# Routing each token tile inside the delta rule, and the experts as a pipeline over tiles

## The chip, the cores and the metric

The kernel runs on one core of a Trainium2 chip. The metric is the device time of one execution in microseconds; the median of three runs is compared. The core has five engines that each take their instructions in order: TensorE (PE; its weight loads are shown as PEld), VectorE (DVE), ScalarE (ACT), GpSimd (POOL) and SyncE (SP, which here only issues DMAs). They meet through semaphores. 16 DMA engines move the data.

## The reference, cut to what matters

Three layers follow each other: a delta-rule attention over 32 heads (4 batches of 8) with 768 time steps, a mixture of eight experts in which every token goes to one, and a dense layer with three input matrices.

```
for t in range(S):                                   # delta rule, S = 768, D = 48
    y[:, :, t] = einsum('bhd,bhde->bhe', q[:, :, t], state)
    v_old = einsum('bhde,bhd->bhe', state, kt)
    state = state + bt * einsum('bhd,bhe->bhde', kt, vt - v_old)
...
e_idx = argmax(x @ w_gate)                           # x: 3072 tokens x 384
for e in range(8):
    mask = e_idx == e
    out[mask] = gate_w * eom * (relu(x[mask] @ w1[e]) @ w2[e])      # 384 -> 1024 -> 384
...
h = maximum(maximum(x @ w1, x @ w2), x @ w3)         # 384 -> 768
out = h @ w_out
```

## The kernel before

The program is a row of blocks, each with one instruction stream per engine.

**Delta rule** (`attention_and_router`). The tokens are 24 tiles of 128 rows: 12 steps k, each with two streams st = 0 and 1 that are worked on side by side. A step is cut into 16 slots, and `walk` writes out by hand, for every engine, what it does in each slot: `CHAIN` is the recurrent part of a step (ks, z, up for each half, then yt and lg: turn the tile round and make its router logits), `INV` is the preparation of a later step (turn the keys, gram, an inversion in levels), `PRE` and `NORM` the normalisation of keys. Stream 1 runs 9 slots behind stream 0. `run` walks w from -1 to 13: in it, a is the step under preparation (k = w), c the step in the chain that began an iteration before, b the one before that, n the next one whose keys are normalised. So four steps are in flight. A bank of PSUM per stream (`chain`) holds all of CHAIN's results; two others and a third (`bank`) those of INV.

The names that matter below: POOL makes `ksq` (NORM part 0), `kn` and `beta_mask` (PRE), `n_lo` ("low") and `n_kb_a` ("kb", which reads the keys in `k_own`); in slot yt it copied the finished tile into `x_all`. SP runs `load_k(k + 1)` and then `load_qv(k)` for each k:

```
for k in range(2, STEPS):
    if k + 1 < STEPS:
        load_k(k + 1, (k + 1) % 2)      # k_raw x2, then k_own x2; k_own of stream st waits for kb_ready[st] >= k
    load_qv(k, k % 2)                   # kq_t and v_in of stream 0, then of stream 1; wait for state_out
```

TensorE's gram of step k and stream 0 (slot 1 of iteration w = k) waits for `qv_in`, that is for kq_t and v_in of this step.

**Routing** (`route_and_sort`). After the last tile, VectorE picks each token's expert from the logits of all 24 tiles at once, TensorE counts (rank of a token among those of its expert), VectorE makes slots and the table of expert ranges, and POOL scatters the 24 tiles with an indirect DMA each into `x_sorted`. The weights of expert 0 are split there in a high and a low part (float32r).

**Experts** (`experts`). 28 tiles of sorted tokens; for each, TensorE does the first layer ("hidden", 18 matmuls of 512 columns into `h_bank`), turns the next tile's x (`transpose_x`, L838), turns h (L859), and does the second layer (24 matmuls of 384 columns into `y_acc`), each engine in a loop from the expert's first tile to its last. VectorE makes the next expert's high parts at an expert's start (`before`), POOL the low parts.

**Last layer** (`last_layer`). Six blocks of 512 tokens; rows are gathered from `y_sorted` with an indirect DMA.

Of the kernel before, what the change touches and what calls it, by code (L numbers as in the profile page):

```python
# [10 lines left out]
I32 = mybir.dt.int32  # L11
# [28 lines left out]
CF_TRI = CF_BASE + C  # L40
CF_ONE = CF_TRI + P
CF_IOTA = CF_ONE + P
CF_STEP = CF_IOTA + E
CF_SUM = CF_STEP + TILES
CF_END = CF_SUM + E * E

# [3 lines left out]
CH_END = CH_REP + U * C  # L50


def constants():
# [11 lines left out]
    cf[:, CF_TRI:CF_TRI + P] = np.arange(P)[:, None] < np.arange(P)[None]  # L65
    cf[:, CF_ONE:CF_ONE + P] = 1.0
    cf[:, CF_IOTA:CF_IOTA + E] = np.arange(E)
    cf[:, CF_STEP:CF_STEP + TILES] = P * np.arange(TILES)
    cf[:, CF_SUM:CF_SUM + E * E] = np.tri(E).reshape(-1)
    ch[:, CH_ID:CH_ID + P] = np.eye(P)  # L70
    ch[:, CH_NEG:CH_NEG + P] = -np.eye(P)
    ch[:, CH_REP:CH_REP + U * C] = np.tile(row == col, (1, U))
    return cf, ch
# [22 lines left out]
def attention_and_router(nc, ctx, sems, kt_in, kh, qh, vh, bh, cf_in, ch_in, wr_in, cf, ch, wr, x_all, logits, xs, ys, xs_zeroed, weights, w1, w2):  # L96
# [36 lines left out]
    y_tile = single("y_tile", [P, X], F32)  # L133
    y_t = single("y_t", [P, KX, P], F32)
    zeros = sb("zeros", [P, X], F32)

# [41 lines left out]
    x_out = pair_of("x_out")  # L178
# [11 lines left out]
    ident_rep = ch[:, CH_REP:CH_REP + U * C]  # L190
    LV0, LVS = 2, LEVELS - 2
# [44 lines left out]
    def _(sp):  # L236
# [24 lines left out]

        sp.wait_ge(zeros_ready, 1)
        with sp.Fori(0, MAXB + 1) as g:
            sp.dma_start(xs[bass.ds(P * g, P), :], zeros[:]).then_inc(xs_zeroed, 16)

        with sp.Fori(TILES, MAXB + 1) as g:
            sp.dma_start(ys[bass.ds(P * g, P), :], zeros[:]).then_inc(xs_zeroed, 16)

# [3 lines left out]
        for k in range(2, STEPS):  # L272
            if k + 1 < STEPS:
                load_k(k + 1, (k + 1) % 2)
            load_qv(k, k % 2)

    @block.tensor
    def _(pe):
# [83 lines left out]
        def chain(k, par, st, what, e):  # L362
            out = yb[st]
            W = 2 * D
            if what == "ks":
# [4 lines left out]
                elif k >= 1:  # L370
                    pe.wait_ge(logit_out[st], k)
# [24 lines left out]
            elif what == "yt":  # L396
# [3 lines left out]
                for c in range(KX):  # L400
                    ins = pe.transpose(out[:, P * c:P * c + P], y_tile[st][:, P * c:P * c + P], ident)
# [863 lines left out]
```

## Time and profile before

| | us |
|---|---|
| median of 3 runs | 1198.79 (1197.86 to 1202.87) |
| profiled execution, its own time | 1203.62 |
| span of the profiled execution | 1201.9 |
| PE busy | 1030.9 (86% of the span) |
| DVE, ACT, POOL busy | 480.0, 365.8, 327.6 |

Busy time is what an engine spends inside instructions. The profile also gives for each stretch of time the granted TensorE clock (PEclk, 1.00 is 2.4 GHz and 0.50 is 1.2 GHz), for each instruction what ended the idle time before it, and for each DMA the time from its issue to its landing.

### The profile page before, as it was taken

To read this page: it belongs to the slowest core of one execution; us is meant where nothing else is said; L and a number is where in the kernel's file an instruction comes from. 1 tells how busy PE (TensorE), PEld (TensorE's weight loads), DVE (VectorE), ACT (ScalarE), POOL (GpSimd) and SP (SyncE) were. 2 spreads that over 40 slices of the span, in tenths; PEclk is the share of its full clock that TensorE was granted. 3 is DMA by queue.
4 is the path that set the end of the run, shared out by engine and by line. 5 is a ranking of instruction groups with operands and counts; after the bars stand their busy time and mean duration, and the time that the engine had idled before them with its cause. 6 is when DMAs were issued, how large, how long until landed. Compare 5 with 4: busy or idle time off the path is not lost. (4 is left out here: it accounts for less than half of the span.)

```text
span 1201.9 us, 31001 instructions
## 1 busy us (share of the span) xinstructions
PE 1030.9 (86%) x13236; PEld 895.3 (74%) x13237; DVE 480.0 (40%) x922; ACT 365.8 (30%) x732; POOL 327.6 (27%) x226
## 2 busy tenths in 40 slices
PE   1699999999999999603988998899959999999999
PEld 1588788888887787502877887788848887888888
DVE  3355555555555554332234323433334233242322
ACT  0245445555545455200212212212222122121211
POOL 2222333232333220084255045531630001000000
PEclk9979999999999999755999999999979999999999
DMA  8712122122111110043333244412320101100000
GB/s 267 270 29 60 29 56 55 43 60 60 29 56 38 40 34 3 1 156 127 138 116 113 85 144 137 144 42 103 111 66 20 45 28 33 33 20 27 7 20 27
DMA packets 59389, 86.29 MB, mean 72 GB/s; under 512 B 29200, under 2 KB 54288, under 8 KB 56720
## 3 DMA queue, kind: packets, MB, share of 16 engines
q1 hardware_dynamic: 53616, 48.46, 12.7%
q0 software_dynamic: 5664, 36.18, 8.9%
q8 instruction: 92, 1.51, 0.5%
q14 instruction: 17, 0.14, 0.0%
HBM read 61.82 MB, written 22.81 MB: 70 GB/s over the span
## 5 line engine op out<-in xcount | busy, mean ns | idle before, releaser
L1009 PE MATMUL hb<-early,last_h 128*128 128x512 f32 x648 | 203.8, 396 | 4.7 <-ACT o_sb L1123 3.6
L1009 PEld LDWEIGHTS hb<-early,last_h 128*128 128x128 f32 x648 | 120.5, 189 | 30.8 <-ACT o_sb L1123 2.7
L1009 PE MATMUL hb<-early,last_l 128*128 128x512 f32 x324 | 126.9, 392 | 0.0
L480 DVE TENSOR_TENSOR p<-bank,cf 128x512 f16<-128x512 f32 x96 | 66.0, 688 | 46.3 <-PE bank L283 46.0
L283 PEld LDWEIGHTS bank<-t,n_hi 64*64 64x64 f16 x2688 | 66.7, 111 | 22.8 <-issue 7.4
L931 POOL TENSOR_TENSOR late<-w_raw,late 128x3072 fp32r<-128x3072 f32 x8 | 59.7, 7459 | 73.6 <-DVE late L918 73.6
L1147 DVE TENSOR_TENSOR m<-hb,m 128x512 f32<-128x512 f32 x36 | 24.9, 692 | 131.4 <-PE hb L1009 131.4
L283 PE MATMUL bank<-t,n_hi 64*64 64x64 f16 x2688 | 72.0, 195 | 5.1 <-issue 4.3
L1009 PE MATMUL ob<-wo_h,early 128*128 128x384 f32 x288 | 74.2, 335 | 0.0
L881 ACT ACTIVATE h_sb<-h_bank 128x512 f32<-128x512 f32 x28 | 16.8, 598 | 186.5 <-PE h_bank L792 186.5
L792 PE MATMUL y_acc<-early,ht_h 128*128 128x384 f32 x240 | 63.4, 345 | 11.3 <-DVE ht_l L903 11.3
L1009 PEld LDWEIGHTS hb<-early,last_l 128*128 128x128 f32 x324 | 61.2, 189 | 13.1
L585 POOL COPY x_all<-y_tile 128x384 f32<-128x384 f32 x24 | 12.1, 505 | 209.9 <-ACT y_tile L451 209.9
L477 DVE TENSOR_TENSOR t<-bank,cf 128x512 f16<-128x512 f32 x72 | 49.8, 692 | 47.9 <-PE bank L283 47.2
L1042 POOL DMA_INDIRECT rows<-y_sorted,idx x24 | 23.1, 962 | 156.3 <-DVE scaled L1137 153.0
L931 POOL TENSOR_TENSOR early<-w_raw,early 128x3072 fp32r<-128x3072 f32 x6 | 44.8, 7463 | 72.7 <-DVE early L918 72.6
L431 ACT CAST t<-bank 128x512 f16<-128x512 f32 x96 | 56.3, 586 | 26.9 <-PE bank L283 24.9
L792 PE MATMUL y_acc<-late,ht_h 128*128 128x384 f32 x208 | 54.0, 340 | 9.7 <-DVE ht_l L903 9.7
L489 DVE TENSOR_TENSOR rhs<-v_in,chain 64x192 f32<-64x192 f32 x96 | 33.4, 348 | 67.9 <-PE chain L374 66.5
L907 DVE COPY y_sb<-y_acc 128x384 f32<-128x384 f32 x28 | 15.6, 558 | 112.2 <-PE y_acc L792 112.2
L792 PE MATMUL h_bank<-early,xt_h 128*128 128x512 f32 x180 | 57.5, 401 | 1.5 <-DVE xt_l L894 1.5
L838 PE MATMUL xt_bank<-cf,x_in 128*128 128x128 f32 x87 | 14.6, 277 | 51.3 <-DMA x_in<-x_sorted 51.3
(157 smaller groups left out, 2258.8 us busy)
## 6 DMA issues: line engine op xcount, KB each, us to landing
w_raw<-w POOLq DMA_DIRECT2D x14, 1536.0 KB, 6.9
kq_t<-qh SPq DMA_DIRECT2D x24, 256.0 KB, 3.3
x_sorted<-zeros SPq DMA_DIRECT2D x32, 192.0 KB, 1.9
x_in<-x_sorted SPq DMA_DIRECT2D x29, 192.0 KB, 2.3
y_sorted<-y_sb SPq DMA_DIRECT2D x28, 192.0 KB, 1.9
k_raw<-kt_in SPq DMA_DIRECT2D x24, 192.0 KB, 3.3
k_own<-kh SPq DMA_DIRECT2D x24, 192.0 KB, 3.3
v_in<-vh SPq DMA_DIRECT2D x24, 192.0 KB, 3.5
```

What stands on the lines that cost most here:

```text
L283: ins = pe.matmul(out[s, C * u:C * u + C], lhs(s, u), rhs(s, u), start=first and u == 0, stop=True, skip_group_check=True)
L431: act.copy(t16[st][:], tb).then_inc(t_out[st], 1)
L477: dve.tensor_tensor(t16[st][:], pb, mask_of(None), ALU.mult).then_inc(jacobi_out[st], 1)
L480: dve.tensor_tensor(p16[st][:], pb, mask_of(lv), ALU.mult).then_inc(prod_out[st], 1)
L489: dve.tensor_tensor(rhs[st][s, :, hh, :], v_in[par][st][s, e], by_head[0:C, hh], ALU.subtract).then_inc(rhs_out[st], 1)
L792: ins = pe.matmul(out, a[x], b[y], start=first and i == 0, stop=last and i == 2)
L881: act.activation(h_sb[:, 0:512], h_bank[0][:, :], ACT.Relu).then_inc(h_out[0], 1)
L907: dve.tensor_copy(y_sb[:], y_acc[:, 0:X]).then_inc(y_out, 1)
L931: pool.tensor_tensor(splits[par][i][1], weights.flat_raw(i), splits[par][i][0], ALU.subtract).then_inc(weights.lo_ready[i], 1)
L1009: ins = pe.matmul(out, a[x], b[y], start=first and i == 0, stop=last and i == 2, skip_group_check=True)
L1042: pool.indirect_dma_start(rows[t][:], None, ys, bass.IndirectOffsetOnAxis(ap=idx[:, t:t + 1], axis=0)).then_inc(rows_got[t], 16)
L1147: dve.tensor_tensor(m1[f % 2][:], h_bank[f % 2][1][:, :], m0[f % 2][:], ALU.max).then_inc(m1_out, 1)
```

## The change

The routing block is gone. In its place, in the delta rule:

- CHAIN gets three more entries. In "lg", VectorE adds four dependent small operations that pick the tile's experts. In "rank", TensorE adds two small matmuls. In "slot", VectorE makes each token's row. In "send", POOL scatters the tile with an indirect DMA from `y_tile`, which is now double. Each expert has a fixed area of 24 tiles in `x_sorted`, so a row's place is known without the other tiles.
- In `walk` the chain of b comes before that of c in each slot, and "ks" of a stream waits for "slot" of its last tile.
- The areas must be zero: 24 writes of 1.5 MB, two for each step, stand in SP's stream behind `load_qv(k)`, each waiting for the one before to land. Before, 32 writes of 192 KB (and 8 of `y_sorted`) stood ahead of the loop.
- The split of expert 0's weights is cut in six pieces, in NORM parts 10 to 12 of steps 2 to 7.
- After the walk, one matmul and eight small VectorE operations make the table of the experts' tiles.

The experts become a pipeline: the second layer of a tile runs in the next tile, half of it ahead of h's transposes and half behind. The outer loop over experts is written out, with each expert's first tile apart. The gates are worked out beside the first tile.

```diff
-    CHAIN = {0: ("ks", 0), 2: ("z", 0), 4: ("up", 0), 6: ("ks", 1), 8: ("z", 1), 10: ("up", 1), 12: ("yt", 0), 14: ("lg", 0)}
-    NORM = {1: [0], 2: [1], 3: [2], 5: [3], 6: [4], 7: [5], 8: [6], 9: [7, 8], 10: [9]}
+    CHAIN = {0: ("ks", 0), 2: ("z", 0), 4: ("up", 0), 6: ("ks", 1), 8: ("z", 1), 10: ("up", 1), 12: ("yt", 0), 14: ("lg", 0),
+             15: ("rank", 0), 16: ("slot", 0), 17: ("send", 0)}
+    NORM = {1: [0], 2: [1], 3: [2], 4: [10], 5: [3], 6: [4], 7: [5], 8: [6], 9: [7, 8], 10: [9], 12: [11], 13: [13], 14: [12]}
...
-                for of, off in ((a, 0), (c, SLOTS), (b, 2 * SLOTS)):
+                for of, off in ((b, 2 * SLOTS), (c, SLOTS), (a, 0)):
...
+        def zero_area(i):
+            if i >= 1:
+                sp.wait_ge(area_zeroed, 16 * i)
+            sp.dma_start(areas[i], zeros[:].unsqueeze(1).broadcast_to((P, E, X))).then_inc(area_zeroed, 16)
...
             load_qv(k, k % 2)
+            zero_area(2 * k - 2)
+            zero_area(2 * k - 1)
...
                 elif k >= 1:
-                    pe.wait_ge(logit_out[st], k)
+                    pe.wait_ge(routed[st], 5 * k - 1)
...
+            elif what == "rank":
+                pe.wait_ge(chosen_ready[st], k + 1)
+                if 2 * k + st >= 1:
+                    pe.wait_ge(counted_ready, 2 * k + st)
+                pe.sem_inc(passed_pe, 1)
+                pe.matmul(out[:, X + P - E:X + P], tri16, chosen[:, 2 * k + st, :], start=True, stop=False, skip_group_check=True)
+                pe.matmul(out[:, X + P - E:X + P], ones16, counted[:], start=False, stop=True,
+                          skip_group_check=True).then_inc(rank_done[st], 1)
...
+            elif what == "slot":
+                to = 2 * k + st
+                dve.wait_ge(rank_done[st], k + 1)
+                dve.tensor_tensor(place[st][:], yb[st][:, X + P - E:X + P], chosen[:, to, :], ALU.mult).then_inc(routed[st], 1)
+                dve.wait_ge(routed[st], 5 * k + 4)
+                dve.tensor_reduce(slot_f[:, to:to + 1], place[st][:], AX.X, ALU.add).then_inc(routed[st], 1)
+                dve.wait_ge(routed[st], 5 * k + 5)
+                dve.tensor_copy(rows_at[:, to:to + 1], slot_f[:, to:to + 1]).then_inc(slot_ready[st], 1)
+                dve.tensor_tensor(counted[:], counted[:], chosen[:, to, :], ALU.add).then_inc(counted_ready, 1)
...
-            if what == "yt":
-                pool.wait_ge(y_out[st], 2 * k + 2)
-                pool.tensor_copy(x_all[:, 2 * k + st, :], y_tile[st][:]).then_inc(x_out[st], 1)
+            if what == "send":
+                to = 2 * k + st
+                pool.wait_ge(slot_ready[st], k + 1)
+                pool.wait_ge(area_zeroed, 16 * (to + 1))
+                if k >= 1:
+                    pool.wait_ge(rows_sent[st], 16 * k)
+                pool.indirect_dma_start(xs, bass.IndirectOffsetOnAxis(ap=rows_at[:, to:to + 1], axis=0),
+                                        y_tile[par][st][:], None).then_inc(rows_sent[st], 16)
...
+        def tile(e, par, g, first):
+            if first:
+                pe.wait_ge(weights.lo_ready[0], e + 1)
+            hidden(par, g)
+            transpose_x(g + 1)
+            if first and e == 0:
+                transpose_h(g)
+                pe.wait_ge(weights.lo_ready[1], 1)
+                return
+            of = 1 - par if first else par
+            pe.wait_ge(ht_lo[1], g)
+            output(of, 0)
+            transpose_h(g)
+            output(of, 1).then_inc(y_done, 1)
+            if first:
+                pe.wait_ge(weights.lo_ready[1], e + 1)
```

POOL's stream at the turn from step 1's keys to step 2, before. `n_kb_a_11` is "kb" of an odd step and stream 1 (here step 1), `ksq` and `kn` belong to the next keys.

```order
L585 COPY x_all<-y_tile_0 128x384 [waits y_out0]
L573 TENSOR_TENSOR n_lo_1<-n_kb_a_11,n_hi_1 128x512 [waits n_hi_ready1]
L593 TENSOR_TENSOR ksq<-k_raw1 128x768 [waits norm_step,k_in1]
L579 TENSOR_TENSOR n_kb_a_11<-k_own_11,beta_k1 128x8x48 [waits beta_k_ready,k_own_in1]
L564 TENSOR_TENSOR kn_01<-k_raw0,nrm 128x8x48 [waits kt_done1,inv_norm]
L569 TENSOR_TENSOR beta_mask_1<-cf,beta 128x1024 [waits gram_out1]
```

The same place of the changed kernel:

```order
L688 TENSOR_TENSOR n_lo_1<-n_kb_a_11,n_hi_1 128x512 [waits n_hi_ready1]
L713 TENSOR_TENSOR ksq<-k_raw1 128x768 [waits norm_step,k_in1]
L704 DMA x_sorted<-y_tile_00,rows_at 28544x384 [waits area_zeroed,slot_ready0]
L694 TENSOR_TENSOR n_kb_a_11<-k_own_11,beta_k1 128x8x48 [waits beta_k_ready,k_own_in1]
L679 TENSOR_TENSOR kn_01<-k_raw0,nrm 128x8x48 [waits kt_done1,inv_norm]
L684 TENSOR_TENSOR beta_mask_1<-cf,beta 128x1024 [waits gram_out1]
```

The copy of a tile that waited only for the tile is gone, and the scatter of stream 0's tile of the step two before, which waits for `slot_ready0`, stands ahead of "kb" of stream 1.

SP's stream at the same turn (k = 2), in the changed kernel; the numbers behind a name are the buffer's parity and the stream.

```order
L274 DMA k_raw1<-kt_in 128x384 [waits kn_ready1]
L278 DMA k_own_10<-kh 128x384 [waits kb_ready0]
L278 DMA k_own_11<-kh 128x384 [waits kb_ready1]
L284 DMA kq_t_00<-qh 128x8x64 [waits state_out0]
L285 DMA v_in_00<-vh 128x384
L284 DMA kq_t_01<-qh 128x8x64 [waits state_out1]
L285 DMA v_in_01<-vh 128x384
L298 DMA x_sorted<-zeros 128x8x384 [waits area_zeroed] x2
```

Only the last row is new; the loads stand in the order in which they stood before, with q and v of stream 0 behind the k_own that waits for "kb" of stream 1.

## Rows read from the trace of the kernel before

**Rows 1.** The page's 40 equal slices: PE's busy tenths, granted clock.

```profile
PE   1699999999999999603988998899959999999999
PEclk9979999999999999755999999999979999999999
```

**Rows 2.** Busy time by stretch: engines, PEclk, DMA share, GB/s.

```profile
56.80:59.40 2.60, 0.04 (x4) 0.00 (x0) 0.00 (x0) 0.09 (x1) 0.38 (x1) 1.00 0.15 54
59.40:73.60 14.20, 12.73 (x191) 11.20 (x190) 5.00 (x9) 4.76 (x10) 6.46 (x6) 0.52 0.20 58
...
178.00:357.00 179.00, 172.26 (x4268) 150.99 (x4267) 101.49 (x233) 96.07 (x205) 58.10 (x55) 1.00 0.18 51
...
501.50:560.50 59.00, 3.24 (x28) 2.77 (x28) 17.54 (x32) 2.75 (x5) 30.69 (x26) 0.50 0.40 138
560.50:873.00 312.50, 282.95 (x1484) 247.28 (x1484) 113.49 (x156) 61.81 (x112) 131.95 (x34) 0.99 0.32 110
```

**Rows 3.** Timeline, last logits to first expert tile: start, length, engine, line, what.

```profile
501.35 0.17 DVE L501 COPY logits<-chain 128x16 f32<-128x16 f32 x1 [3.32 <-PE chain L407]
...
504.59 2.23 PE L726 MATMUL rank<-chosen,counting 128*128 128x192 f16 x24
...
510.13 0.18 DVE L695 CAST slots<-slot_f 128x24 uint32<-128x24 f32 x1
...
511.27 1.99 POOL L741 DMA_INDIRECT x_sorted<-x_all,slots  x1 [12.68 <-DVE slots L695]
511.37 3.44 DVE L706 CAST early<-w_raw 128x3072 fp32r<-128x3072 f32 x2
...
547.99 0.97 POOL L741 DMA_INDIRECT x_sorted<-x_all,slots  x1 [0.30 <-issue]
555.77 0.33 SPq L818 DMA_DIRECT2D x_in<-x_sorted  x1
...
560.54 1.19 PE L792 MATMUL h_bank<-early,xt_h 128*128 128x512 f32 x2 [1.51 <-DVE xt_l L894]
```

**Rows 4.** The page's group of the expert tiles' last operation.

```profile
L907 DVE COPY y_sb<-y_acc 128x384 f32<-128x384 f32 x28 | 15.6, 558 | 112.2 <-PE y_acc L792 112.2
```

**Rows 5.** Timeline of the last expert tile, in the same form.

```profile
861.74 0.56 DVE L907 COPY y_sb<-y_acc 128x384 f32<-128x384 f32 x1 [4.01 <-PE y_acc L792]
...
866.50 0.42 PEld L859 LDWEIGHTS ht_bank<-cf,h_sb 128*128 128x128 f32 x4 [0.26 <-DVE h_sb L899]
...
867.95 0.30 PEld L792 LDWEIGHTS y_acc<-late,ht_h 128*128 128x128 f32 x2 [1.02 <-ACT ht_h L885]
...
872.54 0.56 DVE L907 COPY y_sb<-y_acc 128x384 f32<-128x384 f32 x1 [4.03 <-PE y_acc L792]
```

**Rows 6.** Timeline of one delta-rule step around gram of stream 0 (L318).

```profile
285.30 1.96 PE L318 MATMUL bank<-kq_t 48*64 48x128 f32 x32
...
313.05 0.83 POOL L579 TENSOR_TENSOR n_kb_a<-k_own,beta_k 128x384 f32<-128x384 f32 x1
...
314.28 1.48 SPq L251 DMA_DIRECT2D kq_t<-qh  x1
...
315.80 0.66 SPq L252 DMA_DIRECT2D v_in<-vh  x1
...
318.76 0.73 DVE L489 TENSOR_TENSOR rhs<-v_in,chain 64x192 f32<-64x192 f32 x2 [0.37 <-PE chain L374]
...
319.72 1.13 PE L374 MATMUL chain<-state,kq_t 128*128 128x96 f32 x8
320.78 1.96 PE L318 MATMUL bank<-kq_t 48*64 48x128 f32 x32
```

**Rows 7.** The page's DMA issues: count, KB each, us to landing.

```profile
v_in<-vh SPq DMA_DIRECT2D x24, 192.0 KB, 3.5
```

**Rows 8.** Timeline of SP's stream at the start.

```profile
15.50 24.25 SPq L264 DMA_DIRECT2D x_sorted<-zeros  x32
```

**Rows 9.** Busy time by stretch, at the end of the delta rule.

```profile
480.00:483.50 3.50, 3.50 (x48) 2.86 (x43) 0.66 (x2) 1.07 (x2) 0.00 (x0) 0.52 0.02 5
```

More of the change, by code:

```diff
@@ L93, in rows_in_order, with attention_and_router @@
     return np.ascontiguousarray(out.reshape(BATCH // 2, SEQ // P, 2, P, X).swapaxes(1, 2)).reshape(N, X)
-def attention_and_router(nc, ctx, sems, kt_in, kh, qh, vh, bh, cf_in, ch_in, wr_in, cf, ch, wr, x_all, logits, xs, ys, xs_zeroed, weights, w1, w2):
+def attention_and_router(nc, ctx, sems, kt_in, kh, qh, vh, bh, cf_in, ch_in, wr_in, cf, ch, wr, routing, xs, ys, weights, w1, w2):
     def sem(name):
@@ L132, in attention_and_router @@
     z = single("z", [P, NP, 2, D], F32)
-    y_tile = single("y_tile", [P, X], F32)
+    y_tile = double("y_tile", [P, X], F32)
     y_t = single("y_t", [P, KX, P], F32)
     zeros = sb("zeros", [P, X], F32)
+    best = sb("best", [P, 2], F32)
+    score = single("score", [P, E], F32)
+    top = sb("top", [P, 2], F32)
+    place = single("place", [P, E], F32)
+    rows_at = sb("rows_at", [P, TILES], U32)
+    counted = sb("counted", [P, E], F16)
+    more = sb("more", [P, E, TILES], F32)
+    blocks = sb("blocks", [P, E], F32)
+    sums = sb("sums", [P, E, E], F32)
+    ends = sb("ends", [P, E], F32)
+    begins = sb("begins", [P, E], F32)
+    logits, chosen, slot_f, shift, table = routing
     bank = [[ctx.enter_context(nc.psum_tensor(f"bank{st}{i}", [P, 512], F32)) for i in range(3)] for st in range(2)]
@@ L593, in norm @@
                 pool.tensor_tensor(ksq[:], keys, keys, ALU.mult).then_inc(squares, 1)
+            elif part == 13 and k == STEPS - 2:
+                for i, w in enumerate((w1, w2)):
+                    pool.wait_ge(weights.lo_ready[i], 1)
+                    pool.dma_start(weights.raw[i][:], w[1]).then_inc(weights.raw_again[i], 16)
         pool.wait_ge(const_in, 64)
@@ L746, in experts @@
-def experts(nc, ctx, sems, cf, table, xs, ys, weights, w1, w2, w_in, w_out):
+        for st in range(2):
+            pool.wait_ge(rows_sent[st], 16 * STEPS)
+def experts(nc, ctx, sems, cf, routing, gate, slots, xs, ys, weights, w1, w2, w_in, w_out):
     def sem(name):
@@ L768, in experts @@
     y_sb = sb("y_sb", [P, X])
+    logits, chosen, slot_f, shift, table = routing
+    lg, og = logits[:, :, 0:E], logits[:, :, E:2 * E]
+    best_of = sb("best_of", [P, TILES])
+    spread = sb("spread", [P, TILES, E])
+    exps = sb("exps", [P, TILES, E])
+    picked = sb("picked", [P, TILES, E])
+    denom = sb("denom", [P, TILES])
+    z_gate = sb("z_gate", [P, TILES])
+    exp_gate = sb("exp_gate", [P, TILES])
+    product = sb("product", [P, TILES])
+    moved = sb("moved", [P, E])
     h_bank = [ctx.enter_context(nc.psum_tensor(f"h_bank{i}", [P, 512], F32)) for i in range(2)]
@@ L884, in body @@
                 act.wait_ge(ht_done[n], g + 1)
+                if n == 1 and not (first and e == 0):
+                    act.wait_ge(y_done, g)
                 act.copy(ht[0][:, 4 * n:4 * n + 4].rearrange("p c t -> p (c t)"), ht_bank[n][:, :]).then_inc(ht_hi[n], 1)
+        act.wait_ge(gate_step, 3)
+        act.activation(exps[:], spread[:], ACT.Exp).then_inc(exps_ready, 1)
+        act.wait_ge(gate_step, 4)
+        act.activation(exp_gate[:], z_gate[:], ACT.Exp, scale=-1.0).then_inc(exps_ready, 1)
         split_x(0)
-        of_experts(act, body)
+        of_experts(act, tile)
     @block.vector
@@ L921, in _ @@
+        dve.memset(y_sb[:], 0.0).then_inc(y_out, LEAD)
+        dve.memset(best_of[:, 0:1], 0.0).then_inc(xt_done, 1)
+        dve.wait_ge(xt_done, 1)
+        gates_first()
         split_x(0)
-        of_experts(dve, body, before)
+        gates_last()
+        total = of_experts(dve, tile)
+        output(total)
     @block.gpsimd
```

414 lines of the change are left out of this document (200 added, 214 removed).

## The prediction

> **What bounds the kernel now.** I read the slices of the page first. PE is nine tenths busy or more nearly everywhere, with one hole in slices 17 to 19, where its clock falls too [rows 1]. The table by stretch then gives each stage its limit [rows 2]. In the delta rule (178 to 357) PE is busy 172.3 of 179.0 us at full clock: PE-bound, with DVE at 57% and POOL at 32%. From 501.5 to 560.5 PE does 3.2 us of work in 59. In the experts it is busy 283 of 312.5; in the last layer (slices 31 to 40) every slice is at nine tenths or more [rows 1]. So a gain can come from the hole, from the 10% that PE idles in the experts, and from nothing in the last layer; any delay that reaches PE in the delta rule is paid in full.
>
> **The hole: -42 us.** From the last logits copy (501.35) to the first expert matmul (560.54) there are 59.2 us [rows 3]. What is left of that chain: the logits copy takes 0.17 us, and dependent small DVE operations follow each other at about 0.21. Copy and four operations: 1.0; two rank matmuls with the handovers: 0.6; three operations to the row numbers: 0.6; from there 0.96 to the scatter's start, as from slots (510.31) to 511.27. So the last scatter starts 3.1 us behind the logits. Before, 7.8 us lie from the last scatter's start (547.99) to the first load of x (555.77), and 4.8 from there to the first matmul. The table (nine operations) is ready in the shadow of the scatter's landing. SP must now read two table entries ahead of its first load: no row isolates that, and I put it between 0 and 2, at 1.4. Sum 17.1, a gain of 42. The first split, 24 x_all copies and all full-width routing operations go with the hole; the gates lie beside x's load and the first 6 us of matmuls.
>
> The Trainium skill (DMA: Bandwidth & Descriptors, Latency and other measured facts) gives a table read a floor of about 0.6 us; two would be 1.2, and the sum would be better by 0.2. No row here shows one alone.
>
> **The experts: -40 us.** A plain tile takes 872.54 - 861.74 = 10.80 us, in which PE waits 0.26 for h and 1.02 for its split [rows 5]; 9.52 is work. In the new order the x transposes and 12 matmuls of the tile before stand ahead of h's transposes, and its other 12 and the next hidden part ahead of the next use of ht, so both waits have over 2 us of cover. ACT's second copy waits for y_done, but half a tile passes before PE wants it. DVE's high parts (3.44 us for two [rows 3]) stood ahead of h's maximum; now one stands at a tile's start, 1.7 us in the 4 that hidden takes, and one behind ht_lo. Before, 312.0 us pass from 560.54 to the last y copy for 28 tiles [rows 3 to 5]. New: 28 x 9.52 = 266.6, 2.5 for the first matmuls at half clock (PEclk is 0.50 to 560.5 [rows 2]), 1.5 to drain the last tile, 1.4 for the written-out code at eight expert starts (a guess between 0 and 8): 272. Gain 40, at least 30.
>
> **The delta rule: the term that decides.** POOL's stream has the scatter of stream 0's tile ahead of "kb" of stream 1, and SP's stream has q and v of stream 0 behind the k_own that waits for this "kb". Rows 6 show the old chain: kb 313.05 to 313.88, kq_t issued 314.28, v_in 315.80, landing 3.5 us later at 319.3 [rows 7]; gram starts at 320.78, straight behind ks. The margin is 1.5 us, and it exists only because POOL could run some three slots ahead of the others. The new wait ends that. slot_ready of stream 0 comes behind DVE's rhs (318.76 + 0.73, moved 0.25 by the rank matmuls: 319.74) and three small operations: 320.37. Scatter start +0.96, its length 0.97 [rows 3], kb 0.83, handover and k_own 0.40, kq_t 0.6 (1.5 in this row): v_in is issued at 324.1 to 325.0 and lands at 327.6 to 328.5. PE would be at gram at 321.0. It waits 6.6 to 7.5 us; I take 6.8. Behind gram stands everything of PE, and so of all engines: nothing hides it, and since slot_ready moves with PE, it comes again each step. Steps 2 to 10 have both a scatter and a k_own ahead of q and v (step 11 loads no more keys): 9 x 6.8 = 61.
>
> The clock: PE idle for 2.6 us at 56.8 is followed by 14.2 us at half clock with gram among them, while a stretch at 480 was at half for 3.5 us only [rows 2, 9]. Work at half clock costs half its length: 1.7 to 7.1 us for each wait. Gram, which stands in the longer row, is the first thing after the wait, but what follows is denser than at 60: 3.5 each, 32 in all. The Trainium skill (TensorE: Matmul & The Clock Gate, HAM oscillation) describes a loop whose every round starts cold after a DMA wait; it would make all nine fall. The row at 57 is one gap of 2.6 us, so it can't show that.
>
> Smaller terms. Rank matmuls: 24 in 2.23 us gives 0.09 each [rows 3], with the semaphore 0.2 a tile, 5 us on the PE-bound path. DVE's four routing operations (0.84 us) fall between PE results where DVE idles in one stream, and push one product in the other; the 18 split pieces (0.3 to 0.6 us each) may push others: 6, between 0 and 20. Zeroing: 32 writes of 192 KB took 24.25 us [rows 8], so an area takes 6 and, with its receipt, two take 16 us of a step of 35.5 (285.30 to 320.78 [rows 6]) on a mostly idle DMA (share 0.18); k_raw behind them still lands some slots early, so 0 for the loads. But PE's gap at 56.8 came in the middle of a group of matmuls with the DMA just full of weights: twelve such bursts may open others, 5 us, between 0 and 30. The start gains: the weights now go ahead by 15 us, and gap and half clock at 57 to 73 should go: -7, between 0 and -10. The scatter is 1 us shorter or longer with what DVE does (1.99 beside the casts), in the bounds.
>
> **The sum.** 61 + 32 + 5 + 6 + 5 - 7 = +102 for the delta rule, -42 and -40: +20. The profiled execution took 1203.6 and its like would take 1224; the median of the runs is 4.8 lower, so 1219. About 0.5% (6 us) is what a measurement of this kernel can tell from no change.
>
> **The rivals.**
> - *The wait is there, the clock comes back soon.* Break-even is at (82 - 9) / 9 = 8.1 us for each of the nine waits, where 9 is the smaller terms together. With 6.6 of waiting and 1.7 of clock it is 8.3: time 1201, within the noise. For it: the stretch at 480. Against: gram stands first, and kq_t's issue is sometimes 1.5. 18%, from 1187 to 1206.
> - *No wait, the other side.* If POOL's scatter does not hold back kb, or the loads are early enough in some way that the rows don't show, the gains stand nearly alone: -82 + 9 = -73, time 1126; if a wait of 3 us remains without a drop of clock, 1153. The point is a delay under 1.5 us from 319.3. I find nothing that gives it: the order, not a length, makes the wait, and even a scatter of no length leaves 5 us. But four steps in flight may settle in an order that I don't see. 17%, below 1187.
> - *Worse: the clock stays low, or the zeroing starves PE.* With 7.1 us of half clock at each wait, 32 become 64; with PE gaps at each burst +20 more: 1251 to 1271. For it: 57 to 73 is the only row with a long gap and gram behind it. The Trainium skill (DMA: Bandwidth & Descriptors, Issuing engines are not separate DMA queues) has all queues interleave on the same 16 engines, so that the scatter and the zeros would lengthen the loads at hand; by the rows the zeros are through by then. 13%, above 1245.
> - *The forecast*, 1206 to 1245: 52%.
>
> **Numbers.** Slower by over 0.5% (above 1205): 65%. Within: the upper part of the first rival, 12%. Faster: 23%. The likeliest case alone: 1206 to 1245. For eight in ten I leave out what is under 1150 and over 1262.
>
> **What the profile after would show.** The load of kq_t for stream 0 behind each scatter; PE's gram waiting on a DMA of v_in or kq_t, nine times, 6 to 8 us each, and PEclk at 0.5 behind them; a step of 46 us for the 35.5 of before. The stretch from last logits to first expert matmul about 17 us. y copies 9.5 us apart, with no PE wait at h or ht. PE busy in the last layer as before. I am wrong if gram starts straight behind ks, as at 320.78: then the whole gain stands. If it waits, but PEclk stays at 1, the time is near 1190. If tiles take 10.8 us still, it is up to 40 us more.

## The result, and the profile after

The changed kernel takes **1255.95 us** (median of 4 runs, 1242.3 to 1261.0), the kernel before 1200.83 in the same session: a ratio of 1.042, 95% interval 1.033 to 1.051. It is slower, by 55 us at the medians; the forecast was 1219. The time lies outside the likeliest case (1206 to 1245) and inside the bounds for eight in ten (1150 to 1262). The ratio is one of mean times and leaves out the slowest run, which is why it is below the 1.046 of the medians. The profiled execution is that slowest one, 1261.0 us with a span of 1259.2, against 1203.6 and 1201.9 before, so that the two traces differ by 57.3 us.

First the slices of its page, then busy time by stretch, cut at the first and last logits copy, the first expert matmul and the last y copy:

```profile
PE   1786778878778878798759999999959999999999
PEclk9998887888778889899859999999979999999999
```

```profile
92.20:636.30 544.10, 431.99 (x9034) 378.30 (x9026) 250.84 (x688) 206.90 (x439) 126.57 (x112) 0.86 0.34 111
636.30:650.40 14.10, 1.28 (x7) 0.79 (x7) 5.64 (x26) 2.25 (x4) 0.97 (x1) 0.50 0.14 43
650.40:923.00 272.60, 270.98 (x1483) 245.40 (x1484) 117.65 (x164) 63.05 (x112) 129.08 (x34) 0.99 0.37 128
```

The delta rule, which had nearly every slice at nine tenths [rows 1], now stands mostly at seven or eight with a clock at seven to nine; the hole of 59 us is down to one dent; the experts are solid. With the same cuts in both traces:

| us | before | after | difference | predicted |
|---|---|---|---|---|
| start to first logits copy | 97.4 | 92.2 | -5.2 | -7 |
| first to last logits copy | 403.9 | 544.1 | +140.1 | +109 |
| last logits copy to first expert matmul | 59.2 | 14.1 | -45.1 | -42 |
| experts, to the last y copy | 312.0 | 273.1 | -38.9 | -40 |
| last layer | 329.4 | 335.7 | +6.3 | 0 |

Both gains came as forecast. The loss in the delta rule is 31 us larger, and the last layer, which the change does not touch, became slower too.

**The hole**, in the timeline after (start, length, engine, line, what), answers to [rows 3]:

```profile
636.28 0.17 DVE L555 COPY logits<-chain 128x16 f32<-128x16 f32 x1 [3.32 <-PE chain L449]
638.15 0.15 DVE L572 CAST rows_at<-slot_f 128x1 uint32<-128x1 f32 x1
638.58 0.97 POOL L704 DMA_INDIRECT x_sorted<-y_tile,rows_at  x1 [8.94 <-DVE rows_at L572]
645.56 0.39 SPq L806 DMA_DIRECT2D x_in<-x_sorted  x1
650.38 1.19 PE L785 MATMUL h_bank<-early,xt_h 128*128 128x512 f32 x2 [1.25 <-DVE xt_l L907]
```

The scatter starts 2.3 us behind the logits (forecast 3.1), x's load 7.0 behind that, the first matmul 4.8 behind the load.

**The delta rule.** PE's waits from 60 to 600 (us in all, times, longest us; the largest groups):

```profile
PE bank L360 <- issue: 61.0, 12, 6.3
PE bank L325 <- issue: 27.2, 14, 3.3
PE bank L325 <- DVE t L530: 3.8, 11, 0.8
PE chain L416 <- issue: 3.2, 1, 3.2
PE chain L435 <- issue: 3.2, 1, 3.2
PE chain L449 <- issue: 2.2, 1, 2.2
...
```

L360 is gram: the forecast wait is there, though the profile calls it "issue" and does not name a DMA; that it is v_in follows from the timeline below, and from the first two experiments. But L325, the small matmuls that depend on DVE and ACT, waits 27 us for "issue", that is for nothing that the profile shows. Before, such waits of the same line (L283 there) came to 7.7 us from 97 to 501:

```profile
PE bank L283 <- issue: 7.7, 9, 1.5
```

These are two different stalls, and the timeline tells them apart. The first, around 364:

```profile
364.72 0.15 DVE L572 CAST rows_at<-slot_f 128x1 uint32<-128x1 f32 x1
365.15 1.01 POOL L704 DMA_INDIRECT x_sorted<-y_tile,rows_at  x1 [9.02 <-DVE rows_at L572]
366.19 0.84 POOL L694 TENSOR_TENSOR n_kb_a<-k_own,beta_k 128x384 f32<-128x384 f32 x1
367.06 0.33 SPq L278 DMA_DIRECT2D k_own<-kh  x1
368.03 0.66 SPq L285 DMA_DIRECT2D v_in<-vh  x1
371.41 0.91 PE L360 MATMUL bank<-kq_t 48*64 48x128 f32 x6 [5.72 <-issue]
```

Each row starts within 0.3 us of the end of the one that it waits for, to v_in's issue; 3.4 us behind that PE may go on, at half speed. There are nine such waits, 5.7 to 6.3 us, 53.7 in all, 52.2 us apart (forecast: a step of 46). The second stall, with SP's stream beside it:

```profile
114.87 7.24 SPq L298 DMA_DIRECT2D x_sorted<-zeros  x2
120.06 0.19 PE L325 MATMUL bank<-t,n_hi 64*64 64x64 f16 x2
123.44 0.41 PE L325 MATMUL bank<-t,n_hi 64*64 64x64 f16 x14 [3.19 <-issue]
128.38 0.39 PE L325 MATMUL bank<-tt,p 64*64 64x64 f16 x14
131.57 0.26 PE L325 MATMUL bank<-tt,p 64*64 64x64 f16 x2 [2.81 <-issue]
```

PE stops between the second and the third of sixteen like matmuls, whose operands are all there, while two writes of 1.5 MB of zeros are under way. What it lacks are the instructions themselves. The page lists a DMA queue of their own for them, "q8 instruction: 98, 1.61, 0.5%": 98 packets of 16 KB. The trace has a time for each of these packets; I took each one between 60 us and the last logits, with the share of time that the 16 engines were busy in the 2 us before it, and the PE gap of over 1.2 us that it lies in or within 1.2 us ahead of (the nine long gram waits left out):

```
fetches in all                                79
with the engines over 70% busy before it      22, of which 17 in a gap (41 us)
with less                                     57, of which  1 in a gap (1.6 us)
```

Seventeen of these 18 gaps are of 1.6 to 3.3 us, 41.8 in all, 43.0 with the last. In 17 of the 18, PE goes on 2.2 to 2.5 us after the fetch's packet starts, in the other 3.1; and in 15 the packet starts 5.8 to 7.8 us behind the issue of a write of zeros, that is when that write comes to its end. Nearly no fetch costs anything unless zeros are being written. In the kernel before, the same count finds 13 of 78 fetches with busy engines, and 1 of them in a gap, of 1.5 us. PE's idle time in this stage grew by 85 us, from 26.8 to 112.1; the two stalls are 97 us, so that all other waits together became 11 shorter.

### The profile page after: what moved, and what is told of

It is laid out like the page before. It is cut to its first block and busy times, and to the rows that moved or that the text cites. A ratio compares the mean times of both kernels' runs of the same rounds, so it can differ in the third digit from the quotient of the medians.

```text
span 1259.2 us, 30897 instructions
## 1 busy us (share of the span) xinstructions
PE 1075.4 (85%) x13260; PEld 938.5 (75%) x13260; DVE 516.6 (41%) x1132; ACT 366.9 (29%) x730; POOL 308.2 (24%) x202
## 3 DMA queue, kind: packets, MB, share of 16 engines
q8 instruction: 98, 1.61, 0.5%
## 5 line engine op out<-in xcount | busy, mean ns | idle before, releaser
L360 PE MATMUL bank<-kq_t 48*64 48x128 f32 x768 | 71.0, 356 | 62.0 <-issue 61.0
L360 PEld LDWEIGHTS bank<-kq_t 48*64 48x64 f32 x768 | 63.1, 185 | 64.7 <-issue 64.4
L325 PEld LDWEIGHTS bank<-t,n_hi 64*64 64x64 f16 x2688 | 71.6, 117 | 33.1 <-issue 19.0
L704 POOL DMA_INDIRECT x_sorted<-y_tile,rows_at x24 | 24.4, 1017 | 280.0 <-DVE rows_at L572 280.0
L325 PE MATMUL bank<-t,n_hi 64*64 64x64 f16 x2688 | 76.7, 201 | 11.7 <-issue 10.9
L526 DVE TENSOR_TENSOR n_kb_a<-bank,beta_mask 128x512 f32<-128x512 f32 x48 | 33.1, 690 | 93.8 <-PE bank L360 92.9
L987 POOL TENSOR_TENSOR late<-w_raw,late 128x3072 fp32r<-128x3072 f32 x8 | 54.4, 6797 | 58.4 <-DVE late L925 58.2
L688 POOL TENSOR_TENSOR n_lo<-n_kb_a,n_hi 128x512 f16<-128x512 f32 x24 | 27.7, 1156 | 161.6 <-ACT n_hi L478 161.6
L499 ACT COPY z<-chain 64x192 f32<-64x192 f32 x96 | 29.9, 311 | 122.6 <-PE chain L425 121.3
L894 ACT CAST ht_h<-ht_bank 128x512 fp32r<-128x512 f32 x56 | 32.9, 587 | 109.8 <-PE ht_bank L848 55.5
L325 PE MATMUL bank<-tt,p 64*64 64x64 f16 x1920 | 55.2, 199 | 9.0 <-issue 8.7
L435 PE MATMUL chain<-z,n_kb_a 128*128 128x96 f32 x384 | 59.8, 303 | 3.2 <-issue 3.2
```

Source lines behind the costliest of these rows:

```text
L325: ins = pe.matmul(out[s, C * u:C * u + C], lhs(s, u), rhs(s, u), start=first and u == 0, stop=True, skip_group_check=True)
L360: ins = pe.matmul(out[s, P * p:P * p + P], kq[r, NP * e + p, 0, :], kq[r, NP * e + p, :, :], start=p == 0, stop=True, skip_group_check=True)
L435: ins = pe.matmul(out[:, W * p:W * p + W], n_kb_a[par][st][:, NP * e + p, 1:3, :].rearrange("q a t -> q (a t)"), z[st][:, p].rearrange("q ...
L499: act.copy(z[st][half[hh], :, hh, :], by_head[0:C, hh]).then_inc(z_out[st], 1)
L526: dve.tensor_tensor(n_kb_a[par][st][:, us, 0:3:2, :], x[:, :].rearrange("p (n a i) -> p n a i", n=NP, a=2), beta_mask[st][:, us], ALU.mult ...
L894: act.copy(ht[0][:, 4 * n:4 * n + 4].rearrange("p c t -> p (c t)"), ht_bank[n][:, :]).then_inc(ht_hi[n], 1)
```

## The experiments

Two causes were to be told apart: **A**, the order (scatter ahead of kb ahead of SP's k_own ahead of q and v), and **B**, the zeros ahead of PE's instruction fetches. All ratios are against the kernel before, run on the same chip in the same minutes. The stage times are read as in the table above, from one profiled execution of each kernel; that can lie off the median (kb_first 1176.5 us, both_few 1139.2, the changed kernel 1261.0).

| kernel | A | zeros | median us | ratio (95%) | first to last logits | last layer |
|---|---|---|---|---|---|---|
| changed kernel | yes | 1.5 MB each | 1255.95 | 1.042 (1.033 to 1.051) | 544.1 | 335.7 |
| kb_first | no | same | 1185.08 | 0.987 (0.982 to 0.992) | 462.2 | 335.1 |
| qv_first | no | same | 1185.26 | 0.982 (0.976 to 0.988) | 473.7 | 335.2 |
| zero_few | yes | 6 areas only | 1215.82 | 1.012 (1.007 to 1.017) | 494.9 | 335.1 |
| both_few | no | 6 areas only | 1148.84 | 0.957 (0.952 to 0.962) | 423.4 | 335.3 |
| kb_zero_twice | no | twice 1.5 MB | 1212.29 | 1.011 (1.006 to 1.016) | 487.1 | 335.1 |
| kb_padB | no | 1.5 MB each | 1179.34 | 0.984 (0.980 to 0.988) | 463.0 | 336.4 |
| spread4_padA | no | 384 KB, SP waits | 1193.92 | 0.995 (0.993 to 0.998) | 475.4 | 335.4 |
| spread8_padAB | no | 192 KB, SP waits | 1309.35 | 1.089 (1.083 to 1.095) | 584.9 | 336.0 |
| zero_only_pad80 | yes | 384 KB, ACT | 1207.47 | 1.007 (1.004 to 1.011) | 484.8 | 335.4 |
| act_zero_kbqv | no | 384 KB, ACT | 1148.43 | 0.955 (0.952 to 0.957) | 429.2 | 335.4 |
| act_zero_place | no | 384 KB, ACT | 1143.01 | 0.951 (0.946 to 0.957) | 431.5 | 329.2 |
| act_zero_right | no | 384 KB, ACT | 1138.42 | 0.947 (0.942 to 0.952) | 429.5 | 329.8 |

### Undo A, in two ways

kb_first moves the scatter one slot, behind kb of the other stream:

```diff
-             15: ("rank", 0), 16: ("slot", 0), 17: ("send", 0)}
+             15: ("rank", 0), 16: ("slot", 0), 18: ("send", 0)}
```

> POOL's scatter of a tile moves one slot later, so that kb of stream 1 stands ahead of it; all else is as in the changed kernel. Theory (the scatter holds back kb, kb holds back SP's k_own, and that the loads of q and v for gram): the nine gram waits of 5.7 to 6.3 us go, 54 us, and most of the half clock behind them, 25 to 35: about 1175 against 1256. The 17 PE gaps of 1.6 to 3.3 us that stand beside the writes of zeros stay. Rival (gram's q and v are late because the zeros or the scatter's own transfer slow the loads down): the gram waits stay at 5 us or more, time 1245 to 1256.

qv_first leaves POOL's order alone and changes SP's:

```diff
-                load_k(k + 1, (k + 1) % 2)
+                load_k_raw(k + 1, (k + 1) % 2)
             load_qv(k, k % 2)
+            if k + 1 < STEPS:
+                load_k_own(k + 1, (k + 1) % 2)
```

> SP issues q and v of a step ahead of the next step's k_own, so that it does not wait for kb before them; POOL's order is as in the changed kernel. Theory: the same as with kb first, gram waits gone, 1170 to 1185, unless k_own is then late for kb. Rival (kb or the scatter itself is what gram waits for, by another way than SP's order): gram waits stay, about 1256.

Both took 1185 us, 10 above the 1175 of the one expectation and at the upper end of the other. The same place in kb_first's timeline:

```profile
177.96 1.28 POOL L694 TENSOR_TENSOR n_kb_a<-k_own,beta_k 128x384 f32<-128x384 f32 x1
179.26 0.33 SPq L278 DMA_DIRECT2D k_own<-kh  x1
180.23 0.66 SPq L285 DMA_DIRECT2D v_in<-vh  x1
185.31 0.15 DVE L572 CAST rows_at<-slot_f 128x1 uint32<-128x1 f32 x1
185.74 1.01 POOL L704 DMA_INDIRECT x_sorted<-y_tile,rows_at  x1 [6.50 <-DVE rows_at L572]
```

v_in is now issued 5.1 us ahead of the row numbers; in the changed kernel it stood 3.3 us behind them. Gram's nine long waits are gone in both; kb_first keeps three of 1.3 to 3.4 us and qv_first one of 3.4, each at a fetch. The other stall stays, with gaps of up to 5.2 us in qv_first. That two edits at different links of one chain give the same time shows that it is this chain, and not the length of any transfer in it. The PE waits of kb_first for "issue", from 60 to 553, the largest groups (waits for DVE stood between them):

```profile
PE bank L325 <- issue: 21.5, 19, 3.3
PE bank L360 <- issue: 7.5, 3, 3.4
...
PE chain L435 <- issue: 5.7, 2, 3.4
PE chain L416 <- issue: 4.3, 3, 2.2
...
```

They are spread over whatever matmul happens to be next: a stall of the stream, not of a buffer. Every one over 1.5 us has a fetch packet in it or just ahead.

### Undo B alone, undo both, double B

zero_few and both_few write zeros to areas 0 to 5 of 24 only; the tiles of these inputs lie in no other. That is for these inputs, no general kernel.

```diff
         def zero_area(i):
+            if i >= FEW:
+                return
```

> Only areas 0 to 5 are set to zero (9 MB instead of 36): the writes of zeros end in step 3, and the expert tiles of these inputs read no further area. The order of kb and the scatter is as in the changed kernel. Theory (an instruction fetch of PE stands behind the zeros on the DMA engines): no PE gap inside a group of matmuls from step 4 on, 13 of 17 gone, 32 us, and about 15 of half clock behind them: about 1210; the nine gram waits stay at 5.5 to 6.5 us. Rival (the gaps come from the scatters or from the fetches as such): gaps stay, 1250 to 1256. Second rival (the zeros also make gram's loads late): gram waits shrink to 3 to 5 us, below 1200.

> kb ahead of the scatter, and only areas 0 to 5 set to zero (9 MB instead of 36; these inputs read no further area). Theory: both causes are separate and add up: 1256 - 81 - 46 = about 1130, the delta rule at 36 to 37 us a step as before the change. Rival (with one stall gone another takes its place: the rank matmuls, the routing on DVE, the split pieces): 1145 to 1170, with PE waiting for DVE.

kb_zero_twice writes each area twice.

> kb_first with every area written twice, 72 MB: the second write changes no value. Theory (each fetch of PE's instructions that falls into a write of zeros costs 1.3 to 3.5 us of PE time and some half clock): twice as many fetches are hit, gaps of 65 to 80 us in all instead of 37, time 1215 to 1240 against 1185. Rival (the gaps come from something else that happens twice a step): 16 gaps as in kb_first, 1185.

Busy time from first to last logits copy in zero_few, both_few and kb_first (columns as in [rows 2]):

```profile
91.90:586.90 495.00, 406.50 (x9034) 355.79 (x9026) 252.03 (x688) 206.30 (x439) 126.69 (x112) 0.90 0.21 65
```

```profile
92.10:515.60 423.50, 383.05 (x9034) 333.65 (x9028) 255.20 (x688) 206.64 (x439) 128.66 (x111) 0.98 0.25 76
```

```profile
91.60:553.80 462.20, 402.79 (x9030) 350.09 (x9022) 252.43 (x688) 207.17 (x439) 128.46 (x111) 0.93 0.40 130
```

Undoing A is worth 71 us at the medians, B alone 40, both 107: nearly the sum (by the ratios 67, 36 and 103). With both gone the clock is back at 0.98 and PE busy is 383.1 against 377.2 before:

```profile
97.40:501.40 404.00, 377.16 (x9002) 329.31 (x9002) 210.71 (x483) 206.42 (x439) 109.74 (x108) 0.99 0.15 41
```

both_few's 1149 is not the 1130 of the theory, and lies in the range of its rival. Of what the rival names, the rank matmuls are there, with DVE's choice ahead of them (8 to 9 us, worked out below), and PE's waits for DVE's p and t are as before. The rest that the trace shows are five gaps at fetches, 11.7 us, three of them at the areas that are still written.

In zero_few gram is L363, and its waits are as they were (nine long ones, 52.5 us):

```profile
PE bank L363 <- issue: 54.1, 11, 6.3
```

Behind step 3 no gap is left inside a group of matmuls but one of 1.4, one of 1.3 and one of 1.4 us. The second rival, that the zeros make gram's loads late, falls. kb_zero_twice came at 1212, just below the expected range (1215 to 1240), and its gaps far below (65 to 80 us expected): 19 gaps at fetches, 43 us, for 15 and 35 in kb_first. They did not double, but neither did the fetches that find the engines over 70% busy: 45 for 31, of which 18 and 15 lie in a gap. Beside these stands a gram wait of 10.7 us, where SP's two k_own loads take 8.5 us: with four such writes in a step its loads come late too.

### Shorter writes, and who issues them

spread4_padA and spread8_padAB cut each area into four or eight writes, each behind the landing of the one before (shown for four):

```diff
-            if i >= 1:
-                sp.wait_ge(area_zeroed, 16 * i)
-            sp.dma_start(areas[i], zeros[:].unsqueeze(1).broadcast_to((P, E, X))).then_inc(area_zeroed, 16)
+            for part in range(PARTS):
+                if i >= 1 or part:
+                    sp.wait_ge(area_zeroed, 16 * (PARTS * i + part))
+                sp.dma_start(areas[i][:, 2 * part:2 * (part + 1)], zeros[:].unsqueeze(1).broadcast_to((P, 2, X))).then_inc(area_zeroed, 16)
```

> kb ahead of the scatter as in kb_first; all 36 MB are set to zero, but each area in four writes of 384 KB, each behind the landing of the one before. Beside that 64 bytes of padding behind cf, which shift all later tiles of SBUF. Theory (what a fetch waits for is what is outstanding ahead of it on the DMA engines, so a quarter of the length gives a quarter of the wait): the PE gaps of the delta rule fall from 16 of 1.3 to 3.5 us to under 10 us in all, delta rule at 425 to 440 us from first to last logits (kb_first 462), time 1145 to 1160. Rival (the engines' occupation counts, not the length of a write): gaps as in kb_first, 1185. The padding: if the 128x512 matmuls of the last layer go 0.233 us apart instead of 0.228 because of where their operands lie, the last layer takes 329 instead of 335; if not, 335.

> As spread4_padA, but each area in eight writes of 192 KB, and another 64 bytes of padding behind the early weights, so that early and last tiles lie as in the kernel before, modulo 128 bytes. Theory: gaps as small or smaller; but 16 writes a step at some 2.3 us (landing and issue) are 37 us, as long as the step itself, so that SP comes late to the loads of k: a step of 38 to 40 us, 1165 to 1190. Rival: the loads have slack enough, 1140 to 1155. The last layer at 329 if the place of its operands counts.

My time for spread4 was wrong (1194 for 1145 to 1160), and for spread8 far off (1309 for at most 1190). The gaps at fetches did shrink, but gram (L362) waits again. spread4's waits of the two lines:

```profile
PE bank L362 <- issue: 40.7, 10, 6.9
PE bank L327 <- issue: 7.6, 14, 1.3
```

SP's stream says why. First spread4, then spread8:

```profile
296.30 5.77 SPq L300 DMA_DIRECT2D x_sorted<-zeros  x3
302.11 1.03 SPq L275 DMA_DIRECT2D k_raw<-kt_in  x2
303.19 5.12 SPq L279 DMA_DIRECT2D k_own<-kh  x2
308.95 0.66 SPq L286 DMA_DIRECT2D v_in<-vh  x1
```

```profile
275.43 34.60 SPq L300 DMA_DIRECT2D x_sorted<-zeros  x16
310.07 0.92 SPq L275 DMA_DIRECT2D k_raw<-kt_in  x2
311.04 4.81 SPq L279 DMA_DIRECT2D k_own<-kh  x2
316.50 0.66 SPq L286 DMA_DIRECT2D v_in<-vh  x1
```

In spread8 SP stands in its waits for 34.6 us of a step. k_raw comes late, so ksq, the norms and beta_k, so kb, so k_own, so q and v: gram waits 11 to 24 us each, nine times. The waits' own cost was right (16 at 2.2 us); that the keys' loads are at the head of the chain to gram I had left out, as in the forecast, where k_raw "still lands some slots early".

The zeros therefore move to ACT's queue: one 384 KB write every second slot, eight a step, with a wait only for the area of a step earlier (the first two areas stay with SP at the start).

```diff
+    for p in range(4):
+        INV[4 * p] = INV[4 * p] + [("zero", p)]
+        INV[4 * p + 1] = INV[4 * p + 1] + [("zero", 4 + p)]
...
+            elif what == "zero" and k >= 1 and lv // 4 == st:
+                p = lv % 4
+                if p == 0:
+                    act.wait_ge(area_zeroed[st], 16 + 64 * (k - 1))
+                act.dma_start(areas[2 * k + st][:, 2 * p:2 * p + 2], zeros[:].unsqueeze(1).broadcast_to((P, 2, X))).then_inc(area_zeroed[st], 16)
```

> kb ahead of the scatter; all areas are set to zero, but from ACT's queue, in eight writes of 384 KB a step that stand two slots apart in the order and that nobody waits for within an area, so that SP's queue holds loads only. Theory (a fetch waits for what stands ahead on the DMA engines; spread4 only moved the stall into SP's queue): the PE gaps fall under 10 us in all and no gram wait comes back; ACT pays some 0.4 us for each issue, 3 us of its idle half; delta rule 425 to 435 us from first to last logits, time 1140 to 1155. Rival (ACT's issues delay the copies that PE waits for): 440 to 460, 1160 to 1180. Beside that early and last tiles lie at exactly the addresses of the kernel before (320 bytes of padding, the routing tiles moved to the other end of SBUF): if the place of the operands makes the last layer's matmuls slower, it takes 329 us and not 335.

> As act_zero_place but without the moved tiles, and SP issues q and v ahead of the next step's k_own besides. Theory: the wait for kb is no longer on the path, so that this adds nothing: 1145 to 1161, last layer 335. Rival (k_own, now last in SP's order, comes late for kb): PE waits in the chain, 1165 or more.

> The scatter stands ahead of kb as in the changed kernel; only the zeros are moved to ACT's queue in writes of 384 KB, all areas. Theory: nine gram waits of 5.5 to 6.5 us and their half clock stay, the gaps at the fetches go: about 1256 - 71 + ... taken from the runs so far, act_zero with kb first 1149 plus 71 = about 1215 to 1220. Rival (the gram wait needs the long zeros too): gram waits of 0 to 4 us, below 1190. Beside that 320 bytes of padding put the early tiles at the address that they have in the kernel before, and the last tiles 2112 bytes behind theirs: last layer 329 us if the address of early counts, 335 if not.

Busy time in act_zero_right and in zero_only_pad80:

```profile
92.60:522.10 429.50, 384.10 (x9030) 332.97 (x9023) 255.68 (x688) 206.59 (x439) 128.49 (x111) 0.98 0.41 136
```

```profile
93.10:578.00 484.90, 400.17 (x9034) 350.33 (x9028) 252.23 (x688) 206.10 (x439) 126.59 (x112) 0.92 0.37 120
```

All 36 MB are written, at the DMA share that kb_first had (0.41 for 0.40), and the delta rule takes 429.5 us, 6 more than with a quarter of the zeros. By the count used above, 22 of 79 fetches find the engines over 70% busy, and 5 of them lie in a gap (10 us); in kb_first it was 15 of 31 (35 us). In spread4, where SP issues the same 384 KB writes one behind the other, it is 2 of 21 (6 us). So busy engines alone do not cost a fetch its time; the length of one write does, by these counts. That fits the start times above, where the fetch's packet came when the write was ending. zero_only_pad80, with A left in, has its nine gram waits (53.4 us) and a time of 1207, below the expected 1215 to 1220: A costs 59 us against act_zero_kbqv. act_zero_place and act_zero_kbqv came in their ranges; moving q and v ahead as well adds nothing (429.2 us for 431.5 from first to last logits).

### The last layer

All new kernels but two had 335 to 336 us in the last layer for 329 before, with the same instructions. The group of its main matmuls (busy, mean ns of one), in the kernel before and in the changed one:

```profile
L1009 PE MATMUL hb<-early,last_h 128*128 128x512 f32 x648 | 203.8, 396 | 4.7 <-ACT o_sb L1123 3.6 <-DVE early L1141 1.2
```

```profile
L1065 PE MATMUL hb<-early,last_h 128*128 128x512 f32 x648 | 208.2, 403 | 4.7 <-ACT o_sb L1179 3.6 <-DVE early L1197 1.2
```

Then in act_zero_right and act_zero_kbqv, from 900 on, where a part of the layer is over:

```profile
L1066 PE MATMUL hb<-early,last_h 128*128 128x512 f32 x480 | 149.7, 393 | 3.0 <-ACT o_sb L1180 3.0
```

```profile
L1074 PE MATMUL hb<-early,last_h 128*128 128x512 f32 x486 | 154.4, 399 | 3.0 <-ACT o_sb L1188 3.0
```

From one such matmul's start to the next it is 0.2276 us before and 0.2332 after: 972 of them make 5.4 us. The change allots SBUF otherwise: the tiles called early (activations) and last (weights) used to lie one behind the other, and the routing tiles, 2112 bytes, now lie between them. I moved them by padding and by allotting the routing tiles from the other end (this is act_zero_place; act_zero_right has it without the pad):

```diff
         cf = sb("cf", [P, CF_END])
+        pad = sb("pad", [P, 80])
...
-        routing = (sb("logits", [P, TILES, 2 * E]), sb("chosen", [P, TILES, E], F16), sb("slot_f", [P, TILES]), sb("shift", [P, E]),
-                   sb("table", [P, 2, E], I32))
+        def right(name, shape, dt=F32):
+            return ctx.enter_context(nc.sbuf_tensor(name, shape, dt, side="right"))
+        routing = (right("logits", [P, TILES, 2 * E]), right("chosen", [P, TILES, E], F16), right("slot_f", [P, TILES]), right("shift", [P, E]),
+                   right("table", [P, 2, E], I32))
```

> kb_first with 64 bytes of padding behind the early weights only: early stays where it is modulo 128 bytes, last moves by 64. If it is the place of the moving operand (early) that counts, the last layer stays at 335; if it is that of the stationary one (last) or the two against each other, it goes to 329. Delta rule and experts as in kb_first, so 1185 or 1179.

> act_zero_place without its 320 bytes of padding: the last tiles lie straight behind the early ones as in the kernel before, but both 320 bytes lower. If the distance between the two operands counts, the last layer takes 329 us; if the address itself does, 335. All else as act_zero_place: 1143 or 1149.

The places, worked out from the order and the sizes in the kernels (bytes in a partition):

| kernel | early, against before | last, against before | between the two | last layer |
|---|---|---|---|---|
| before | 0 | 0 | 0 | 329.4 |
| act_zero_place | -64 | -64 | 0 | 329.2 |
| act_zero_right | -384 | -384 | 0 | 329.8 |
| zero_only_pad80 | -64 | +2048 | 2112 | 335.4 |
| spread4_padA | -320 | +1792 | 2112 | 335.4 |
| spread8_padAB | -320 | +1856 | 2176 | 336.0 |
| kb_padB | -384 | +1792 | 2176 | 336.4 |
| all others | -384 | +1728 | 2112 | 335.1 to 335.7 |

Early lies 384 bytes lower, not 320 as the expectations count: `table` (64 bytes) has also left its place ahead of it. So act_zero_place does not have the addresses of before, but both tiles 64 lower, and kb_padB has both shifted by multiples of 128 bytes; its last layer is the slowest all the same. kb_padB's 1179 us is the number that was expected if the layer went to 329, but the layer did not. act_zero_right's went to 329.8, as expected if the distance counts.

The last layer does not follow early's own address: -64 and -384 each stand with both times. It goes with the distance between the two tiles, but also with last's own address, since no run moved last without the distance. The experts part the two. There the first layer of the even experts multiplies `xt` by early, that of the odd ones `xt` by late, and `xt` and late are allotted behind last and move with it. In the changed kernel the matmuls on early are 0.2331 us apart for 0.2291 before, those on late 0.2283 for 0.2291; in act_zero_right both are at 0.2291. So a tile that moves is not slow by that; the pair of which one tile moved against the other is. Why the distance counts, and which distances are good, the runs don't show.

## Why the prediction was right or wrong

Its direction and its main cause hold; the sum of +20 was 37 short of the traces' 57, and the time fell in the range of the third rival.

- **The hole, -42**: measured -45.1. The scatter's start came 0.28 us behind the row numbers for the 0.96 that I had taken from [rows 3], and from there to x's load it took 7.0 us where it had been 7.8, with two table reads more. Right, 3 us too cautious.
- **The experts, -40**: measured -38.9. The last y copies are 9.53 us apart (forecast 9.52), 28 tiles take 273.1 (272). Right, with some luck: 28 x 9.53 is 266.8, and the rest is 6.3 us for the forecast 5.4, of which 1.4 was a guess.
- **"9 x 6.8 = 61"**: nine waits, steps as named, 53.7 us. The chain of [rows 6] was read rightly; 0.7 of the 0.8 us too much in each is the scatter's start again. kb_first and qv_first show the cause.
- **The clock, "3.5 each, 32 in all"**: the gram waits are followed by 4.7 to 6.9 us at half clock, 52 in all, so 26. Right, a little high; kb_first, without these waits, has PE 29 us less busy. The Trainium skill (TensorE: Matmul & The Clock Gate, HAM oscillation) describes such a loop, cold at each round after a DMA wait; the trace agrees: all nine waits, of 5.7 us and more, were followed by half clock.
- **"rank matmuls 5", "DVE 6 (0 to 20)"**: in both_few, where neither stall covers them, PE is 5.9 us busier than before, rank matmuls included (7.8 us of their own time, partly overlapped), and waits 2.8 us for chosen; its waits for DVE's p and t are 8.0 us as before. So 8 to 9 for the first and 0 for the second.
- **Zeroing, "5 us, between 0 and 30": the step that failed, by size.** The mechanism was named (PE's gap in the middle of a group with the DMA full), but it was priced as an occasional thing. It measured 43 us of gaps, outside the bounds, and most of the other 21 us that PE's busy time grew by half clock (432.0 - 377.2 = 55, less 8 for the rank matmuls and 26 for gram). The forecast priced no clock behind such short gaps: of the 11 of 2.2 to 3.3 us that began at full clock, 10 were followed by half clock, for 3.4 to 10.2 us. What the price left out is a rate: 22 of 79 fetches find the engines busy and 17 of them stall, by 2.4 us on average. [Rows 2] had the gap of 2.6 us at 57 as its one instance, and the trace has a fetch in it, at 57.1, behind 2 us with the engines 99% busy; the count of fetches stood on the page of the kernel before as well, and multiplying the two was the missing step. The Trainium skill (Runtime: NRT & Kernel Launch, Instruction fetch mechanics) says that each sequencer fetches blocks of 16 KB by a DMA queue of its own and that crossing a block is "mostly hidden". The packets of 16 KB agree; mostly hidden holds in the kernel before (1 gap, of 1.5 us, at 78 fetches from 60 to 501) and not beside 1.5 MB writes.
- **"0 for the loads"**: right for the changed kernel as far as the runs tell (gram's waits are the same with a quarter of the zeros), but it had less margin than I thought: spread4 and spread8 use it up.
- **The start, -7**: -5.2.
- **The last layer, "as before"**: +6.3, of which the main matmuls make 5.4, from the place of tiles in SBUF. The forecast had no term for it.
- **The rivals.** "No wait" and "clock comes back soon" are out. "Worse: the clock stays low, or the zeroing starves PE", 13% and 1251 to 1271, holds the time. Of its two parts the starving is true, and larger than it says; the clock is not (3 us a gram wait, not 7). That 1256 lies in its range is in part luck: its 1251 is made of 32 us of clock that did not come. The rows would have borne a higher chance for the starving.

Where the expected gain went: 89 us of gains (hole, experts, start) came, and 140 us went into the delta rule and 6 into the last layer. Of these, 107 us at the medians (act_zero_kbqv against the changed kernel) are the two stalls, and go away without giving up anything of the change.

**The version that beats both** is act_zero_right: kb ahead of the scatter, zeros from ACT's queue in 384 KB writes, last straight behind early as before. 1138.42 us, ratio 0.947 (0.942 to 0.952).

## What to carry to other kernels

When a wait enters an in-order stream, follow every queue behind it to the next one, loads too: here one slot in POOL's order was worth 71 us at the medians. Price background DMA by counting PE's instruction fetches on the page and asking how many will fall under it, cut large writes up, and give them a queue whose waits hold nothing else. And compare stages that the edit didn't touch: if they move, look at where the tiles lie.

## What the runs showed of the hardware that was not expected

- A fetch of PE's instructions (16 KB, 0.9 to 1.9 us of transfer) that found the DMA engines over 70% busy beside 1.5 MB writes mostly stalled PE: 17 of 22 in the changed kernel, for 1.2 to 3.3 us (up to 5.2 in qv_first), in the middle of a group of matmuls, named "issue" in the profile. PE went on 2.2 to 2.5 us after the fetch's packet started. With 384 KB writes at a DMA share of 0.41 it was 5 of 22.
- PE gaps as short as these cost clock too: 10 of 11 of 2.2 to 3.3 us were followed by a granted clock of 0.50 for 3.4 to 10.2 us in the changed kernel.
- A 128x512 fp32r matmul stream ran at 0.2276 or 0.2332 us per matmul with the same instructions, depending on how the two operands' tiles lie to each other in SBUF (0, or 2112 and 2176 bytes between them).
- Sixteen writes of 192 KB, each behind the landing of the one before, take 34.6 us, 2.2 each; 1.5 MB so chained takes 5.6 to 8.6, 7.0 in the middle.
